# Batch 1's attention moved from beside batch 0's value and u products to beside its mix and output products, in a fused attention and two-MLP kernel

## The chip, the cores and the metric

The kernel runs on one core of a Trainium2 chip. The metric is device time in microseconds (us) of one execution. Besides TensorE (PE; its weight loads are listed as PEld) the core has VectorE (DVE), ScalarE (ACT), GpSimd (POOL) and SyncE (SP), each of which takes its instructions strictly in program order and waits for the others through semaphores. SP issues the loads and ACT the stores of the intermediate result.

## The reference, cut to what matters

For 8 batches of 576 tokens: a linear attention (8 heads of 64), then a gated MLP whose gate is mixed over tokens, then a second MLP with a convolution over tokens.

```python
q_s = softmax over the 64 of a head of q        # exp(q - max) / (sum + 1e-9)
k_s = softmax over the 576 tokens of k
kv = einsum('bhsd,bhse->bhde', k_s, v);  x = einsum('bhsd,bhde->bhse', q_s, kv)

h = gelu(x @ w_in);  u, v = halves of h
v_n = (v - mean) / sqrt(var + 1e-6) * g_ln
v_s = einsum('ts,bsd->btd', w_sg, v_n) + b_sg[None, :, None]
x1 = x + (u * v_s) @ w_out

y = (relu(x1 @ w_in2)) * sigmoid(conv over tokens) @ w_out2
```

## The kernel before, in words

The first two stages are run batch by batch in a loop `body(m, a, n)`: the gated MLP of batch m, the attention of batch a = m + 1, and the first steps of batch n = m + 2 (maximum and subtraction for its q and k). The third stage, the second MLP, follows for all batches and isn't touched. Every fp32 product is made of three: an operand is split into a high part, which ACT rounds (`hi_...`), and a low part, which DVE or POOL subtracts (`lo_...`), and PE adds high*high, high*low and low*high. Weights are split the same way, once, from a place in `plain_arena` where the raw weight was loaded, and such places are shared with tiles that are used later.

On PE the order of `body(m, a)` is: value product in four steps of d (`v_part`, 12 matmuls of 512 columns a step) with the last two `x_piece` between them, the value tail, four `u_unit` (24 matmuls of 288 columns each), four `sg_unit` (the mix over tokens, 24 matmuls and 4 of a tail), then `o_part` (the output product) with the next batch's first two `x_piece`. Among these stand the attention of batch a: five `turn_q` (transposes of q, 4 matmuls each) and five `kv_piece` (4 matmuls each).

What runs beside it, for batch m: ACT's `gelu_v`, then DVE's `moments` and `normalise` with POOL's `inverse_deviation`, ACT's `hi_vn`, POOL's `lo_vn`, and a small transfer `move_tail`; this is called the norm chain below. `u_unit(m, 2)` and `(m, 3)` reuse the banks that ACT's `gelu_u(m, 0)` and `(m, 1)` empty, and these stand behind `hi_vn(m, 0)` and `hi_vn(m, 1)` in ACT's order. In the mix, DVE's `affine`, POOL's `gate`, ACT's `hi_g` and DVE's `lo_g` follow one another for each of the four f. For batch a: ACT's `exp_q`, DVE's `sum_q` (a sum, then L1097 and a reciprocal), POOL's `scale_q`, PE's `turn_q`, ACT's `hi_q` and DVE's `lo_q` (`tile(j)`); and the subtraction of the maximum of k, ACT's `exp_k`, `kv_piece`, `finish_kv`, `hi_kv`, `lo_kv`. `max_k` reads a load of k transposed (kT), which `spread_kmax` sends through memory to all partitions.

Batch 0 has no batch before it, so its attention is `first_attention`, and `body(0, 1, 2)` follows it while weights are still being loaded and split.

## Time and profile before

| | |
|---|---|
| Times of three runs | 951.46, 952.41 and 952.91 us, median 952.41 |
| The profiled execution | 951.53 us, of which the span of the trace is 949.7 |
| Busy share of the span | PE 97%, PEld 91%, DVE 64%, ACT 40%, POOL 36% |
| Idle of PE from 28 us to 220 us | three waits, of 2.08, 1.91 and 2.67 us, the last of them ending at 56.88 |
| Chain that ended last | PE 90%, DVE 5%, DMA 1%, issue 1%, ACT 1% |

The busy share is over the whole span. The change lies in its first 125 us, and there the table of slices shows PE at 6 to 9 tenths, beside 9 for nearly all that follows; how long PE waits, and for whom, is read from the timeline of that stretch.

### The profile page before, as it was taken

Reading aid. Unit: us, or ns where it says so; the run is one execution under the profiler, and the core shown is the slowest. Engines: PE = TensorE matmul, PEld = TensorE weight load, DVE = VectorE, ACT = ScalarE, POOL = GpSimd, SP = SyncE. Lnnn points to the kernel's source line nnn. Section 1 sums busy time; section 2 is a strip of 40 time slices with the busy share of each in tenths; the row PEclk is TensorE's granted clock in tenths of the full one; section 3 lists DMA queues with packets and bytes.
Section 4 is the critical chain, followed back from the end, with each engine's and each line's share of the span. In section 5 each row is a group of like instructions: output and inputs, shape, how many; then the busy total and the mean of one; then the engine's idle time right before and its main releaser. Section 6 shows DMA issues by size and latency. Waiting matters only on the chain.

```text
span 949.7 us, 14686 instructions
## 1 busy us (share of the span) xinstructions
PE 925.5 (97%) x5980; PEld 865.6 (91%) x5980; DVE 607.9 (64%) x951; ACT 375.8 (40%) x564; POOL 345.7 (36%) x222
## 2 busy tenths in 40 slices
PE   6689999999999999999999998999999999999998
PEld 6589999899999998999999997999999989999987
DVE  6784765657747656576356797866667676667660
ACT  3561543434524434345224245533434343434331
POOL 4742634446436344464304233322232222232220
PEclk8889999999999999999999999999999999999999
DMA  9805216125062161340312302020202020200001
GB/s 316 272 20 166 91 30 189 50 75 193 12 164 92 32 190 46 80 138 12 132 53 95 110 13 73 12 77 24 78 23 73 23 72 23 82 25 18 29 23 55
DMA packets 50482, 77.84 MB, mean 82 GB/s; under 512 B 4336, under 2 KB 22768, under 8 KB 49520
## 3 DMA queue, kind: packets, MB, share of 16 engines
q1 hardware_dynamic: 45808, 67.48, 22.3%
q10 hardware_dynamic: 4608, 9.44, 2.6%
q8 instruction: 47, 0.77, 0.3%
q14 instruction: 19, 0.16, 0.1%
HBM read 56.97 MB, written 18.89 MB: 80 GB/s over the span
## 4 chain that ended last, share of the span: by engine, by line
PE 90%; DVE 5%; DMA 1%; issue 1%; ACT 1%; POOL 0%; SPq 0%; ACTq 0%; DVEq 0%
PE psum L437 54%; PE psum L429 28%; PE psum L495 4%; PE psum L578 2%; PE psum L471 2%; PE psum L530 1%; DMA plain_arena<-in_q 1%; DVE plain_arena L1291 1%; DVE split_arena L1273 1%; DVE split_arena L1409 0%; DVE plain_arena L1289 0%; PE psum L450 0%; DMA plain_arena<-in_k 0%; DVE plain_arena L1094 0%; DVE plain_arena L1105 0%
## 5 line engine op out<-in xcount | busy, mean ns | idle before, releaser
L437 PE MATMUL psum<-split_arena 128*128 128x288 f32 x4032 | 560.8, 297 | 6.2 <-ACT plain_arena L823 2.7
L437 PEld LDWEIGHTS psum<-split_arena 128*128 128x128 f32 x4032 | 547.3, 189 | 13.0 <-ACT plain_arena L823 3.1
L429 PE MATMUL psum<-split_arena 128*128 128x512 f32 x1248 | 299.1, 394 | 4.6 <-DVE split_arena L1409 2.6
L429 PEld LDWEIGHTS psum<-split_arena 128*128 128x128 f32 x1248 | 232.3, 189 | 52.1 <-DVE split_arena L1409 3.5
L1535 POOL TENSOR_TENSOR plain_arena<-plain_arena 128x576 f32<-128x576 f32 x64 | 107.8, 1684 | 281.2 <-ACT plain_arena L891 281.2
L1294 DVE SCALAR_TENSOR_TENSOR plain_arena<-plain_arena 128x576 f32<-128x576 f32 x64 | 96.2, 1503 | 2.2
L1289 DVE TENSOR_SCALAR plain_arena<-plain_arena 128x576 f32<-128x576 f32 x64 | 36.0, 563 | 90.6 <-ACT plain_arena L885 90.6
L1492 POOL TENSOR_TENSOR plain_arena<-plain_arena 128x576 f32<-128x576 f32 x32 | 46.6, 1455 | 123.3 <-DVE plain_arena L1218 123.3
L885 ACT ACTIVATE plain_arena<-psum 128x576 f32<-128x576 f32 x64 | 41.7, 651 | 105.7 <-PE psum L437 74.6
L891 ACT ACTIVATE plain_arena<-plain_arena 128x576 f32<-128x576 f32 x64 | 43.7, 682 | 42.9 <-DVE split_arena L1409 39.8
L1218 DVE SCALAR_TENSOR_TENSOR plain_arena<-psum,plain_arena 128x576 f32<-128x576 f32 x32 | 26.2, 818 | 53.7 <-PE psum L578 53.7
L1409 DVE TENSOR_TENSOR split_arena<-plain_arena,split_arena 128x576 fp32r<-128x576 f32 x64 | 53.2, 832 | 10.7 <-ACT split_arena L897 9.7
L1291 DVE SCALAR_TENSOR_TENSOR plain_arena<-plain_arena 128x576 f32<-128x576 f32 x64 | 56.0, 874 | 2.3
L1017 ACT ACTIVATE plain_arena<-psum 128x512 f32<-128x512 f32 x36 | 21.4, 595 | 87.5 <-PE psum L429 87.4
L1486 POOL TENSOR_TENSOR split_arena<-plain_arena,split_arena 128x1024 fp32r<-128x1024 f32 (+1 forms) x24 | 48.3, 2026 | 17.8 <-ACT split_arena L835 17.8
L1481 POOL TENSOR_TENSOR plain_arena<-plain_arena 128x2 f32<-128x2 f32 (+1 forms) x24 | 19.6, 818 | 89.3 <-DVE plain_arena L1191 89.3
L1456 POOL TENSOR_TENSOR plain_arena<-plain_arena 128x1024 f32<-128x1024 f32 (+1 forms) x24 | 38.4, 1618 | 35.7 <-DVE plain_arena L1085 35.7
L1461 POOL TENSOR_TENSOR plain_arena<-plain_arena 128x1024 f32<-128x1024 f32 (+1 forms) x24 | 39.6, 1652 | 27.5 <-DVE plain_arena L1100 27.4
L495 PE MATMUL psum<-plain_arena 128*128 128x130 f32 x320 | 44.7, 287 | 2.9 <-ACT plain_arena L770 2.9
L897 ACT ACTIVATE split_arena<-plain_arena 128x576 fp32r<-128x576 f32 x64 | 43.1, 674 | 8.1 <-POOL plain_arena L1535 8.1
L1225 DVE TENSOR_TENSOR split_arena<-plain_arena,split_arena 128x576 fp32r<-128x576 f32 x32 | 24.3, 758 | 33.7 <-ACT split_arena L850 33.7
L495 PEld LDWEIGHTS psum<-plain_arena 128*128 128x128 f32 x320 | 42.4, 203 | 3.0 <-ACT plain_arena L770 3.0
(81 smaller groups left out, 756.9 us busy)
## 6 DMA issues: line engine op xcount, KB each, us to landing
x_dram<-plain_arena ACTq DMA_DIRECT2D x32, 288.0 KB, 2.1
plain_arena<-x_dram SPq DMA_DIRECT2D x8, 1152.0 KB, 5.5
out_rows<-plain_arena SPq DMA_DIRECT2D x36, 256.0 KB, 2.0
plain_arena<-in_v SPq DMA_DIRECT2D x32, 256.0 KB, 3.2
plain_arena<-in_kT SPq DMA_DIRECT2D x7, 1152.0 KB, 9.2
plain_arena<-in_k SPq DMA_DIRECT2D x7, 1024.0 KB, 5.4
plain_arena<-in_q SPq DMA_DIRECT2D x7, 1024.0 KB, 5.7
plain_arena<-in_w_in SPq DMA_DIRECT2D x8, 512.0 KB, 5.6
```

The source lines that it names most:

```text
L429: mm = e.matmul(out, stat[s], mov[m], start=first and n == 0, stop=last and n == 2, skip_group_check=True)
L437: mm = e.matmul(out[:, h, 0:NH], stat[s], mov[m][:, h * NH:(h + 1) * NH], start=first and n == 0, stop=last and n == 2, skip_group_check=True)
L495: mm = e.matmul(kv_sums[:, d // 2, d % 2, 0:VW], kn[:, j, d * P:(d + 1) * P], v_place(b, j)[:, d, :], start=j == 0 and d % 2 == 0, stop=j ...
L885: e.activation(dst, main_sets[f % 2][:, :, 0:NH], ACT.Relu).then_inc(h_relu, 1)
L891: e.activation(gt[:, f % 2, :], cv[:, f % 2, :], ACT.Sigmoid).then_inc(h_gate, 1)
L897: e.activation(hg(0, par, f), gt[:, f % 2, :], ACT.Identity).then_inc(hg_hi, 1)
L1291: e.scalar_tensor_tensor(out=out, in0=h[:, 0:T], scalar=conv[:, f, 0:1], in1=out, op0=ALU.mult, op1=ALU.add).then_inc(conv_chain, 1)
L1294: e.scalar_tensor_tensor(out=out, in0=h[:, 2:T + 2], scalar=conv[:, f, 2:3], in1=out, op0=ALU.mult, op1=ALU.add).then_inc(h_conv, 1)
L1409: e.tensor_tensor(hg(1, par, f), gt[:, f % 2, :], f32(hg(0, par, f)), ALU.subtract).then_inc(hg_lo, 1)
L1486: e.tensor_tensor(vn[1][0:rows, t:t + n, :], vg[0:rows, t:t + n, :], f32(vn[0][0:rows, t:t + n, :]), ALU.subtract).then_inc(vn_lo, 1)
L1492: e.tensor_tensor(uT[:, f, :], uT[:, f, :], tmp[:, f % 2, :], ALU.mult).then_inc(gate_done, 1)
L1535: e.tensor_tensor(gt[:, f % 2, :], gt[:, f % 2, :], hp[:, f % 2, 1:T + 1], ALU.mult).then_inc(hg_full, 1)
```

## The change

In `body(0, 1, 2)` alone, PE no longer has `turn_q(1, 0)` ahead of the value tail, nor `kv_piece` and `turn_q` behind `u_unit(0, 0)` and `(0, 2)`: all ten pieces of batch 1's attention now stand behind `sg_unit(0, 1)`, `(0, 2)` and `(0, 3)`. The exponentials and sums of batch 1 move with them, behind `gelu_u` on ACT and behind `normalise` on DVE; the subtraction of k's maximum moves from DVE (`sub_second_k`) to POOL (`sub_k`). The weights of the mix (`W_SG`) are loaded and split earlier, those of the output (`W_OUT`) later, from other places: `W_SG[1]` from where `w_in` was staged, `W_OUT` from where kT lies, so that the load of batch 2's kT now waits for `lo_w_out`. The first loads of kT, q, k and v of batch 1 come in another order.

```diff
@@ places of the raw weights
-                 for f, at in ((0, UT_AT), (2, UT_AT + 1024))]
+                 for f, at in ((0, KT_AT), (2, KT_AT + 1024))]
-                for j, n, at in ((0, 2, X1_AT), (2, 2, VG_AT + 3 * F), (4, 1, BSG_AT))]
+                for j, n, at in ((0, 2, X1_AT), (2, 2, UT_AT), (4, 1, BSG_AT))]
@@ sync: load_kT
+                if isinstance(b, int) and b == 2:
+                    e.wait_ge(w_out_lo, len(W_OUT))
@@ sync: first loads
+            load_w(W_SG[2], w_sg_raw[2])
+            e.wait_ge(kv_step, NJ - 1)
+            load_w(W_SG[0], w_sg_raw[0])
             load_kT(1)
-            load_w(W_SG[2], w_sg_raw[2])
+            e.wait_ge(w_lo, 2)
+            load_w(W_SG[1], w_sg_raw[1])
+            load_q(1)
+            load_k(1)
...
             spread_kmax(1)
+            for n in range(len(W_OUT)):
+                load_w(W_OUT[n], w_out_raw[n])
@@ tensor: body
                 for f in range(FT):
                     u_unit(m, f)
-                    if f % 2 == 0:
+                    if f % 2 == 0 and not start:
                         kv_and_turn(f // 2)
                 for f in range(FT):
                     sg_unit(m, f)
-                    if f < 2:
+                    if start:
+                        if f == 1:
+                            turn_q(a, 0)
+                            kv_and_turn(0)
+                        elif f == 2:
+                            kv_and_turn(1)
+                            kv_and_turn(2)
+                        elif f == 3:
+                            kv_and_turn(3)
+                            kv_piece(a, NJ - 1)
@@ scalar: body
+                    if start and f >= 2:
+                        hi_late(W_OUT, w_out_raw, w_out_hi, f - 2)
...
+                if start:
+                    for u in range(NU):
+                        exp_q(a, u)
+                    for u in range(NU):
+                        exp_k(a, u)
@@ vector: body
+                if start:
+                    lo_w_out(0)
+                    lo_w_out(1)
+                    sum_q(a, 0)
+                    affine(m, 0)
+                    sum_q(a, 1)
+                    sum_q(a, 2)
+                    lo_g(m, 0)
+                    max_k(n, 0)
+                    affine(m, 1)
+                    tile(0)
+                    tile(1)
+                    lo_g(m, 1)
+                    max_k(n, 1)
+                    affine(m, 2)
+                    tile(2)
+                    tile(3)
+                    lo_g(m, 2)
+                    affine(m, 3)
+                    tile(4)
@@ gpsimd: body
+                if start:
+                    for u in range(NU):
+                        sub_k(a, u)
                 for f in range(FT):
                     gate(m, f)
+                    if start and f == 0:
+                        for u in range(NU):
+                            scale_q(a, u)
```

The order on DVE between the end of the first attention and batch 0's moments (`BN_STATS`), before: `lo_x(0, 3)`, the last `sum_q`, three subtractions of k's maximum (L1117), the split of `W_SG[1]` (L1266) and of `W_OUT` (L1261).

```order
L1160 TENSOR_TENSOR split_arena<-psum,split_arena 128x576
L1094 TENSOR_REDUCE plain_arena<-plain_arena 64x8
L1097 TENSOR_SCALAR plain_arena<-plain_arena 64x8
L1100 RECIPROCAL plain_arena<-plain_arena 64x8
L1117 TENSOR_TENSOR plain_arena<-plain_arena 128x1024 x2
L1117 TENSOR_TENSOR plain_arena<-plain_arena 64x512
L1266 TENSOR_TENSOR split_arena<-plain_arena,split_arena 128x1152
L1261 TENSOR_TENSOR split_arena<-plain_arena,split_arena 128x1024 x2
L1174 BN_STATS plain_arena<-plain_arena 128x6 x2
```

The same stretch now, from `lo_x(0, 0)` (L1191; L1297 splits a piece of `W_SG`, L1159 is `max_k(1, ...)`, L1123 `max_q(1, ...)`):

```order
L1191 TENSOR_TENSOR split_arena<-psum,split_arena 128x576
L1297 TENSOR_TENSOR split_arena<-plain_arena,split_arena 128x576
L1191 TENSOR_TENSOR split_arena<-psum,split_arena 128x576
L1297 TENSOR_TENSOR split_arena<-plain_arena,split_arena 128x1152
L1191 TENSOR_TENSOR split_arena<-psum,split_arena 128x576
L1159 TENSOR_REDUCE plain_arena<-plain_arena 128x2
L1191 TENSOR_TENSOR split_arena<-psum,split_arena 128x576
L1297 TENSOR_TENSOR split_arena<-plain_arena,split_arena 128x1152
L1159 TENSOR_REDUCE plain_arena<-plain_arena 128x2
L1123 TENSOR_REDUCE plain_arena<-plain_arena 128x16 x2
L1123 TENSOR_REDUCE plain_arena<-plain_arena 64x8
L1205 BN_STATS plain_arena<-plain_arena 128x6 x2
```

The sums of q, the subtractions on k and the split of `W_OUT` have left the stretch ahead of batch 0's moments; maxima of k and q, which stood further ahead, now end it, and a 576-wide split stands between the first two `lo_x`.

DVE from the last two `normalise` (L1205) on, before (L1134 is `lo_q`, L1128 `max_k(2, ...)`, L1218 the first `affine`):

```order
L1205 TENSOR_SCALAR plain_arena<-plain_arena 128x512 x2
L1205 TENSOR_SCALAR plain_arena<-plain_arena 64x512
L1134 TENSOR_TENSOR split_arena<-psum,split_arena 128x4x128
L1128 TENSOR_REDUCE plain_arena<-plain_arena 128x2
L1134 TENSOR_TENSOR split_arena<-psum,split_arena 128x4x128
L1128 TENSOR_REDUCE plain_arena<-plain_arena 128x2
L1218 SCALAR_TENSOR_TENSOR plain_arena<-psum,plain_arena 128x576
```

And now, `normalise` being L1236:

```order
L1236 TENSOR_SCALAR plain_arena<-plain_arena 128x512 x2
L1236 TENSOR_SCALAR plain_arena<-plain_arena 64x512
L1292 TENSOR_TENSOR split_arena<-plain_arena,split_arena 128x1024 x2
L1132 TENSOR_REDUCE plain_arena<-plain_arena 128x16
L1135 TENSOR_SCALAR plain_arena<-plain_arena 128x16
L1138 RECIPROCAL plain_arena<-plain_arena 128x16
L1249 SCALAR_TENSOR_TENSOR plain_arena<-psum,plain_arena 128x576
```

The two splits of `W_OUT` (L1292) and the first `sum_q` (L1132 to L1138) now stand ahead of the first `affine` (L1249).

POOL from the last weight split on, before: three `sub_q(1, ...)` (L1456), three `scale_q` (L1461), the norm chain (L1481, L1486), four gates (L1492).

```order
L1456 TENSOR_TENSOR plain_arena<-plain_arena 128x1024 x2
L1456 TENSOR_TENSOR plain_arena<-plain_arena 64x512
L1461 TENSOR_TENSOR plain_arena<-plain_arena 128x1024 x2
L1461 TENSOR_TENSOR plain_arena<-plain_arena 64x512
L1481 TENSOR_TENSOR plain_arena<-plain_arena 128x2 x2
L1486 TENSOR_TENSOR split_arena<-plain_arena,split_arena 128x1024
L1481 TENSOR_TENSOR plain_arena<-plain_arena 64x1
L1486 TENSOR_TENSOR split_arena<-plain_arena,split_arena 128x1024
L1486 TENSOR_TENSOR split_arena<-plain_arena,split_arena 64x512
L1492 TENSOR_TENSOR plain_arena<-plain_arena 128x576 x4
```

And now (L1508 is `sub_q`, L1533 and L1538 the norm chain, L1520 `sub_k`, L1544 `gate`, L1513 `scale_q`):

```order
L1508 TENSOR_TENSOR plain_arena<-plain_arena 64x512
L1533 TENSOR_TENSOR plain_arena<-plain_arena 128x2 x2
L1538 TENSOR_TENSOR split_arena<-plain_arena,split_arena 128x1024
L1533 TENSOR_TENSOR plain_arena<-plain_arena 64x1
L1538 TENSOR_TENSOR split_arena<-plain_arena,split_arena 128x1024
L1538 TENSOR_TENSOR split_arena<-plain_arena,split_arena 64x512
L1520 TENSOR_TENSOR plain_arena<-plain_arena 128x1024 x2
L1520 TENSOR_TENSOR plain_arena<-plain_arena 64x512
L1544 TENSOR_TENSOR plain_arena<-plain_arena 128x576
L1513 TENSOR_TENSOR plain_arena<-plain_arena 128x1024 x2
L1513 TENSOR_TENSOR plain_arena<-plain_arena 64x512
```

`scale_q(1, ...)` has moved from ahead of the norm chain to behind it, and three `sub_k(1, ...)` and a gate stand between.

## Rows read from the trace of the kernel before

**Rows 1.** PE's timeline, 31 to 62 us: start, duration, engine, line, operation.

```profile
31.91 4.07 PE L429 MATMUL psum<-split_arena 128*128 128x512 f32 x12
...
41.61 1.06 PE L437 MATMUL psum<-split_arena 128*128 128x288 f32 x6 [2.08 <-DVE split_arena L1160]
...
47.30 4.62 PE L429 MATMUL psum<-split_arena 128*128 128x512 f32 x12 [1.91 <-DVE split_arena L1160]
...
56.88 4.97 PE L437 MATMUL psum<-split_arena 128*128 128x288 f32 x24 [2.67 <-ACT plain_arena L823]
```

**Rows 2.** Chain of work that ended last, 77 to 122 us: start, duration.

```profile
77.28 0.53 PE psum L578 x4
77.82 0.89 PE psum L495 x8
78.71 0.44 PE psum L471 x4
...
92.54 14.38 PE psum L437 x108
...
121.78 3.18 PE psum L437 x24
```

**Rows 3.** Busy time by stretch, with granted clock (after POOL busy).

```profile
41.60:47.30 5.70, 3.79 (x18) 2.96 (x18) 4.88 (x8) 3.25 (x6) 4.90 (x4) 1.00 0.98 386
47.30:51.80 4.50, 4.50 (x13) 3.53 (x14) 4.43 (x5) 4.29 (x5) 3.25 (x2) 0.62 0.15 63
```

**Rows 4.** DVE's and POOL's timelines, narrow stretches at 49 and 64 us.

```profile
48.80 1.18 DVE L1117 TENSOR_TENSOR plain_arena<-plain_arena 128x1024 f32<-128x1024 f32 x1
...
49.90 2.06 DVE L1117 TENSOR_TENSOR plain_arena<-plain_arena 128x1024 f32<-128x1024 f32 x1
...
48.95 1.93 POOL L1461 TENSOR_TENSOR plain_arena<-plain_arena 64x512 f32<-64x512 f32 x1 [0.33 <-DVE plain_arena L1100]
...
63.87 2.44 DVE L1205 TENSOR_SCALAR plain_arena<-plain_arena 128x512 f32<-128x512 f32 x1
...
63.63 2.40 POOL L1486 TENSOR_TENSOR split_arena<-plain_arena,split_arena 128x1024 fp32r<-128x1024 f32 x1 [1.07 <-ACT split_arena L835]
```

**Rows 5.** POOL's timeline, 24 to 117 us.

```profile
24.14 9.33 POOL L1474 TENSOR_TENSOR split_arena<-plain_arena,split_arena 128x1024 fp32r<-128x1024 f32 x4
...
67.95 3.63 POOL L1486 TENSOR_TENSOR split_arena<-plain_arena,split_arena 128x1024 fp32r<-128x1024 f32 x2 [1.14 <-ACT split_arena L835]
78.83 1.42 POOL L1492 TENSOR_TENSOR plain_arena<-plain_arena 128x576 f32<-128x576 f32 x1 [7.25 <-DVE plain_arena L1218]
...
101.46 6.03 POOL L1468 TENSOR_TENSOR plain_arena<-plain_arena 128x1024 f32<-128x1024 f32 x3
...
110.37 1.91 POOL L1461 TENSOR_TENSOR plain_arena<-plain_arena 128x1024 f32<-128x1024 f32 x1 [1.87 <-DVE plain_arena L1100]
```

**Rows 6.** DVE's timeline, 28 to 101 us.

```profile
28.38 1.34 DVE L1128 TENSOR_REDUCE plain_arena<-plain_arena 128x2 f32<-128x1152 f32 x1
...
56.03 1.27 DVE L1174 BATCH_NORM_STATS2 plain_arena<-plain_arena 128x6 f32<-128x512 f32 x2
...
58.14 0.69 DVE L1134 TENSOR_TENSOR split_arena<-psum,split_arena 128x512 fp32r<-128x512 f32 x1
...
96.44 2.92 DVE L1085 TENSOR_REDUCE plain_arena<-plain_arena 128x16 f32<-128x1024 f32 x3
100.58 0.77 DVE L1242 TENSOR_TENSOR psum<-psum,split_arena 128x576 f32<-128x576 f32 x1 [1.21 <-PE psum L437]
```

**Rows 7.** ACT's timeline, 53 to 69 us.

```profile
53.60 1.28 ACT L823 ACT_TABLE_LOAD   x1
...
67.77 0.63 ACT L843 ACTIVATE plain_arena<-psum 128x576 f32<-128x576 f32 x1
```

**Rows 8.** DMA issues at 84 and 90 us: size, time from issue to landing.

```profile
plain_arena<-in_q SPq DMA_DIRECT2D x1, 1024.0 KB, 5.8
...
plain_arena<-in_kT SPq DMA_DIRECT2D x1, 1152.0 KB, 9.1
```

More of the change, by code:

```diff
@@ L939, in body @@
                 hi_x(m, DT - 2)
+                if late:
+                    exp_k(a, 2)
+                    exp_q(a, 2)
+                hi_x(m, DT - 1)
                 if start:
-                    for u in range(NU):
-                        exp_q(a, u)
-                hi_x(m, DT - 1)
+                    hi_late(W_SG, w_sg_raw, w_sg_hi[1], 1)
                 hi_x_tail(m)
@@ L983, in body @@
                         hi_w2(5)
-                if n is not None:
+                if n is not None and not start:
                     exp_q(n, 0)
@@ L1332, in tile @@
                         lo_q(a, j)
-                if a is not None and not start:
+                if a is not None and not start and not late:
                     sum_q(a, 0)
@@ L1346, in body @@
                         lo_w2(w)
-                if start:
-                    for u in range(NU):
-                        sub_second_k(u)
-                    lo_w_sg(1)
-                    lo_w_out(0)
-                    lo_w_out(1)
                 moments(m, 0)
-                tile(0)
+                if not start:
+                    tile(0)
                 sum_tail(m)
```

124 lines of the change are left out of this document (68 added, 56 removed).

## The prediction

> **What bounds the kernel now.** I read PE's waits first, then its timeline, the chain of waits, the granted clock by stretch, and last DVE's, POOL's and ACT's timelines where PE waits. From 56.88 us on PE has no wait that these views show up to 220 us; the chain runs through PE alone [rows 2]. Ahead of that PE waits three times: 2.08 us ahead of 41.61, 1.91 ahead of 47.30, 2.67 ahead of 56.88 [rows 1]. The first two are for `lo_x`, which stands on DVE behind batch 1's maxima and sums of q; the third is for batch 0's gelu on ACT, which stands behind batch 1's exponentials and the splits of `W_SG[1]` and `W_OUT`. Around them PE is slow as well: 12 matmuls of 512 columns take 4.62 us where the granted clock averages 0.62, and the first u product takes 4.97 where the same 24 matmuls take 3.18 later [rows 1 to 3]. So what there is to win is this front, and since all of PE's work behind it is unchanged, the time moves by as much as the start of batch 0's output product moves, which I call S. Before, S is 92.54: from it run 108 matmuls in 14.38 us, and batch 1's first u product starts at 121.78 [rows 2].
>
> **What goes.** Without the three waits (6.7), the slow clock behind the second (about 1.8) and `turn_q(1, 0)` (0.44), PE would reach batch 0's first u product at about 48.0 [rows 1, 2]. One new wait comes in on the way. POOL splits the four `w_in` from 24.14 in 9.33 us, to 33.47 [rows 5], and `lo_w_sg(2)`, which reads both inputs from SBUF as L1117 does, now stands between the first two `lo_x` on DVE, at 31.8. What such a subtraction does beside POOL the trace shows at 49 us: the first L1117 takes 1.18 us, the next, asked for while POOL's L1461 was waiting, takes 2.06, and that L1461, of half the size, takes 1.93 where the full size takes 1.91 [rows 4, 5]. They take turns, one whole instruction at a time. The Trainium skill says the same (SBUF — State Buffer, Who interferes with whom: such a DVE instruction and a GpSimd one that reads SBUF share a port pair, the loser is fully blocked, and reductions never contend); by it the terms below would be the same. So `lo_w_sg(2)` ends at about 34.2, the second `lo_x` at 34.9, and PE, whose first 6 matmuls of the 12 at 31.91 end near 34.4 [rows 1], loses 0.5. U products then start at 48.4.
>
> **Batch 0's norm chain.** `x_piece(0, 3)` starts where PE's idle time now begins, 39.53, plus 0.5: 40.0. Then about 1.0 for it, 0.65 for `hi_x` (an ACT operation on 576 columns, 0.63 [rows 7]) and 1.1 for the split on ACT (estimate from that, twice the width), so DVE's low split of `W_SG[1]` starts at 42.8; it and `max_k`, 1.3 each, and three `max_q`, 2.92 [rows 6], end at 48.2. The moments start there instead of at 56.03. But now POOL subtracts q's maxima beside them, 46.6 to 51.4 (two full sizes at 1.91 and a half [rows 5]), and the small operations of `moments(0, 0)` with two inputs in SBUF take turns with it: between 1.0 (they all slip in at one boundary, 50.4) and 1.9 (they wait for the end). I take 1.5, so the chain runs as if from 49.7. Its lengths are those of before, counted from 56.03 [rows 4, 5, 7], less 0.6 for the `lo_q` inside (58.14, [rows 6]): `gelu_u(0, 1)` ended at 68.40, so 11.8 on, 61.5; the last `lo_vn` at 71.58, so 14.95 on, 64.65. PE waits for `gelu_u(0, 0)` some 2.4 and for `gelu_u(0, 1)` 1.1, since no attention lies between the u products any more. The fourth ends at 61.5 + 3.2 = 64.7, two mixes of 3.18 + 0.53 [rows 2] at 72.1. Those waits cost nothing beyond what follows, because what follows is later.
>
> **The wait that takes over.** PE at 72.1 wants `turn_q(1, 0)`, hence `scale_q(1, 0)`, and that stands on POOL behind three `sub_k`, 6.03 us, and a gate, 1.42 [rows 5], all of which used to be elsewhere. From 64.65: DVE has `lo_w_out(0)` waiting since 63.6 and takes its turn first, 1.15 (L1117's size, 1.18 [rows 4]); `sub_k` 2.4, to 68.2; `lo_w_out(1)`, 1.15; `sub_k`, to 71.75; L1097 of `sum_q`, 0.1; the last `sub_k`, to 73.1; `affine(0, 0)` ended meanwhile at 73.0; gate, 74.5; another small turn of DVE, 0.1; `scale_q`, 1.91: 76.5. PE has waited 4.4. Why DVE gets the boundary: `normalise` L1205, blocked from 63.87 on by a POOL instruction that ended at 66.03, was done at 66.31, beside POOL's next [rows 4]. From 76.5 PE has five turns (0.44), five `kv_piece` (0.89) and two mixes (3.71), 14.07 in all [rows 2], and S = 90.6. In between I find no further wait: batch 2's kT is loaded only after `lo_w_out`, 69.35, and lands 9.1 later [rows 8], at 78.5; `max_k(2, 0)` and `affine(0, 1)` then end at 81.3 where PE asks at 84.7, `lo_q(1, 0)` at 82.0 where PE asks at 82.9. So S comes 1.95 earlier.
>
> **What is given back.** First the clock. The waits of 1.91 and 2.67 were each followed by a stretch at the low clock that cost 1.8 (4.97 less 3.18), the one of 2.08 was not, with 1.00 granted behind it [rows 1 to 3]. A wait of 4.4 should be: 1.8, bounds 0 and 3.5 (two such stretches). The same behind the wait of 2.4 is swallowed by the next waits. Second, batch 2's q. Its load waits for the last `turn_q(1, ...)`, which stood well ahead of S and now stands 0.9 ahead of it. It goes out at S - 0.5, its small second part at S + 0.1, each lands 5.8 later [rows 8] and a little more for two loads of v in front: S + 6.5. Then `max_q`, 2.92, three pairs of `add_x` (1.5 a pair, from 0.77 an operation) and `lo_x`, 0.7 [rows 6]: S + 14.5, while `x_piece(1, 1)` asks for it at S + 13.6 (14.38 less its own 0.8 [rows 2]). That is 0.9, bounds 0 and 2.7. Before, `max_q` ran at 96.44, S + 3.9, and hid.
>
> Number of activation table loads, stores, all of batches 1 to 7 and the second MLP: unchanged, 0.
>
> **Sum**: -1.95 + 1.8 + 0.9 = +0.75, on the profiled 951.53, so 952.3; the median of before lies 0.9 above its profiled run, so 953.1, which I round to 953.0. Within 0.2% (1.9 us, about what a measurement of this kernel can tell from no change) the change is nothing.
>
> **Rivals.**
> 1. *The stall goes elsewhere but DVE and POOL don't hold each other up much.* If the small operations slip past (t = 48.2 instead of 49.7) and the `W_OUT` splits don't delay `sub_k`, `scale_q(1, 0)` is done 3.8 us earlier, near 72.7, S falls to 86.8, and the sum is -5.7 + 1.8 + 0.9 = -3.0: 949.4. Half of this, -1.1, is as easily had. For it: POOL's and DVE's rows overlap at 101.46 with `add_x` at its full speed [rows 5, 6], so not everything contends. Against: rows 4.
> 2. *POOL wins the boundaries.* Its next instruction is always ready behind `lo_vn`. Then both `lo_w_out` wait for the end of `sub_k` (70.7), and two splits (2.3), `sum_q` with its two small steps (1.6), affine (0.8), gate and scale (3.3) follow one another: 78.8 instead of 76.5, and the sum is +3.0: 955.4. This one is slower. It decides as soon as `sub_k` runs through without a gap: its three instructions in 6.0 us. At a delay of 1.2 beyond my sum the bound is passed. For it: at 49.90 POOL, having asked first, went ahead of DVE [rows 4].
> 3. *The clock stays up, or falls only while PE waits anyway.* Then +0.75 - 1.8 = -1.05: 951.4. For it: 2.08 without a fall.
> 4. *Batch 2's q lands late*, by its upper bound: +0.75 + 1.8 = +2.5: 955.0. Kmax of batch 2 and two v loads go out in the 3 us ahead of it.
> 5. *The change doesn't do what it says*, PE's front still waits as before for q or weights: `W_SG[1]` is issued at 28.9 and wanted at 41.6, q wanted at 45.3, with 5.8 and more to land [rows 8]; against it speaks that slack.
>
> **How the numbers follow.** My forecast 0.45; rival 1, whole or half, 0.25; rival 2 0.13; rival 3 0.09; rival 4 0.06; rival 5 0.02. Faster by over 0.2%: most of rival 1 and a little of rival 3 and of mine, 0.25. Slower: rival 2, rival 4, and the upper end of mine, 0.26. Within: 0.49. Between the whole of rival 1 and rival 2 the range is 949.6 to 955.6; my forecast's own is 951.5 to 954.5.
>
> **What would show it.** In the profile after: no wait of PE from 35 us to about 48, and the first u product there at full clock (3.2 us); waits of some 2.4 and 1.1 ahead of the third and fourth; `lo_w_sg(2)` with 1.6 or more instead of 0.75; one long wait of PE for `scale_q`, 3 to 5 us, ending near 76; `sub_k` stretched to about 8.5; a low clock behind; 108 matmuls starting near 92; batch 1's first u product at 121 to 123. I am wrong if POOL and DVE run through each other there, if the long wait is under 2 us, or if a new one stands between S and batch 1's value product over 3 us.

## The result and the profile after

The changed kernel takes 958.94 us (median of 6 runs, 957.16 to 960.45), the kernel before 952.64 (6 runs, 951.46 to 954.03): a ratio of 1.0065, 95% interval 1.005 to 1.0079. It is slower by 6.3 us. I had forecast 953.0 within 949.6 to 955.6, so the range missed it.

PE's timeline of the changed kernel, 34 to 132 us, with start, duration, engine, line, and the idle time ahead in brackets:

```profile
34.99 1.66 PE L436 MATMUL psum<-split_arena 128*128 128x512 f32 x6 [1.26 <-DVE split_arena L1191]
...
48.08 6.55 PE L444 MATMUL psum<-split_arena 128*128 128x288 f32 x48
57.41 12.50 PE L444 MATMUL psum<-split_arena 128*128 128x288 f32 x72 [2.77 <-ACT plain_arena L859]
...
78.45 1.08 PE L478 MATMUL psum<-plain_arena 128*128 128x128 f32 x4 [4.28 <-POOL plain_arena L1513]
...
95.04 10.63 PE L444 MATMUL psum<-split_arena 128*128 128x288 f32 x78
107.50 6.16 PE L444 MATMUL psum<-split_arena 128*128 128x288 f32 x30 [1.83 <-DVE plain_arena L1280]
...
128.33 3.35 PE L444 MATMUL psum<-split_arena 128*128 128x288 f32 x24
```

The front answers to [rows 1] much as foretold: u products start at 48.08 (I said 48.4), the first 48 matmuls at full clock. Then come three waits: for gelu on ACT (2.77; I said 2.4), for `scale_q(1, 0)` on POOL (4.28; I said 4.4), and for the first `add_x` on DVE (1.83; I said 0.9). That the second is of the size foretold is luck: both its ends are some 2 us later than I had them (74.17 and 78.45, not 72.1 and 76.5). Behind each the clock is down. These are rows of busy time by stretch for PE alone: stretch, its length, PE busy (count), granted clock, DMA share, GB/s.

```profile
57.40:66.50 9.10, 9.10 (x48) 0.67 0.06 14
...
74.10:84.00 9.90, 5.62 (x27) 0.66 0.37 143
...
107.50:113.50 6.00, 5.88 (x30) 0.72 0.45 173
```

The account, by equal rows of the timelines: the output product of batch 0 (S) starts at 95.04, where the same view of the kernel before has 92.38; batch 1's first u product at 128.33 where it has 121.61. So 2.7 us are lost up to S, 4.1 between S and that product, and the rest of the spans' difference (957.7 less 949.7), 1.3, behind it. These are single profiles: the one of the kernel before lies 1.1 under its median, the changed kernel's 0.6 over, so 1.7 of the 8.0 are not in the 6.3 of the medians. Another profile of the same front, of the control e12 below, has S at 94.00.

**Up to S.** What follows PE's long wait took 95.04 less 78.45, 16.6 us, instead of 14.07: 2.5 of clock. The wait itself ended at 78.45, not 76.5, because of what the narrow timelines of DVE and POOL show:

```profile
65.19 5.26 DVE L1292 TENSOR_TENSOR split_arena<-plain_arena,split_arena 128x1024 fp32r<-128x1024 f32 x1 [4.66 <-ACT split_arena L894]
...
64.63 2.38 POOL L1520 TENSOR_TENSOR plain_arena<-plain_arena 128x1024 f32<-128x1024 f32 x1
...
66.98 4.62 POOL L1520 TENSOR_TENSOR plain_arena<-plain_arena 128x1024 f32<-128x1024 f32 x2
```

`lo_w_out(0)` asks at 65.19, while the first `sub_k` runs. That ends at 66.98, and POOL's second goes ahead: DVE gets its turn only at 69.3, ahead of the third and smallest, and is done at 70.45.

**Behind S.** Batch 2's q goes out at 94.58 with k, v and batch 3's kT right behind it (95.80 to 97.77). On DVE `max_q` waits for q, and the third `add_x` waits for a store of batch 0's rows to land, since its place in `x1` is still being read:

```profile
102.93 2.93 DVE L1123 TENSOR_REDUCE plain_arena<-plain_arena 128x16 f32<-128x1024 f32 x3 [4.38 <-DMA plain_arena<-in_q]
...
111.12 0.76 DVE L1280 TENSOR_TENSOR plain_arena<-psum,split_arena 128x576 f32<-128x576 f32 x1 [1.54 <-DMA x_dram<-plain_arena]
```

PE waits 1.83, and the 30 matmuls behind run 6.0 us, to 113.50, where 30 of the 108 in 14.38 [rows 2] would take 4.0. The two sum to 3.8 of the 4.1. The late store (3.6 us to land) hides behind the slow clock here; the experiments bring it out.

**Behind batch 1's first u product** the last 1.3 is clock. Far down PE waits the same time for the same thing in both kernels, and only the changed one's profile has slower rows behind it, a little in the first and most in the second (before, then after):

```profile
577.61 1.66 PE L429 MATMUL psum<-split_arena 128*128 128x512 f32 x6 [1.97 <-DVE split_arena L1409]
579.11 3.61 PE L437 MATMUL psum<-split_arena 128*128 128x288 f32 x24
```
```profile
584.35 1.87 PE L436 MATMUL psum<-split_arena 128*128 128x512 f32 x6 [1.98 <-DVE split_arena L1461]
586.01 4.71 PE L444 MATMUL psum<-split_arena 128*128 128x288 f32 x24
```

### The profile page after: what moved, and what is told of

It is laid out like the page before. It is cut to its first block, busy times and chain, and to the rows that moved or that the text cites. A ratio compares the mean times of both kernels' runs of the same rounds, so it can differ in the third digit from the quotient of the medians.

```text
span 957.7 us, 14686 instructions
## 1 busy us (share of the span) xinstructions
PE 928.5 (97%) x5980; PEld 869.3 (91%) x5980; DVE 614.8 (64%) x948; ACT 375.3 (39%) x564; POOL 351.4 (37%) x225
## 4 chain that ended last, share of the span: by engine, by line
PE 88%; DVE 7%; DMA 2%; issue 1%; POOL 1%; ACT 1%; SPq 0%; ACTq 0%; DVEq 0%
PE psum L444 52%; PE psum L436 28%; PE psum L502 3%; PE psum L478 2%; PE psum L585 2%; PE psum L537 1%; DVE plain_arena L1123 1%; DMA plain_arena<-in_q 1%; DVE plain_arena L1322 1%; DVE split_arena L1304 1%; DVE plain_arena L1205 1%; DVE split_arena L1461 0%; DVE plain_arena L1320 0%; DMA plain_arena<-in_k 0%; PE psum L457 0%
## 5 line engine op out<-in xcount | busy, mean ns | idle before, releaser
L1544 POOL TENSOR_TENSOR plain_arena<-plain_arena 128x576 f32<-128x576 f32 x32 | 46.4, 1451 | 118.7 <-DVE plain_arena L1249 118.7
L1461 DVE TENSOR_TENSOR split_arena<-plain_arena,split_arena 128x576 fp32r<-128x576 f32 x64 | 53.2, 832 | 10.9 <-ACT split_arena L913 10.0
L1249 DVE SCALAR_TENSOR_TENSOR plain_arena<-psum,plain_arena 128x576 f32<-128x576 f32 x32 | 26.1, 815 | 47.4 <-PE psum L585 47.4
L1508 POOL TENSOR_TENSOR plain_arena<-plain_arena 128x1024 f32<-128x1024 f32 (+1 forms) x24 | 38.4, 1618 | 49.0 <-DVE plain_arena L1123 49.0
L1538 POOL TENSOR_TENSOR split_arena<-plain_arena,split_arena 128x1024 fp32r<-128x1024 f32 (+1 forms) x24 | 48.2, 2024 | 17.8 <-ACT split_arena L851 17.8
L814 ACT ACTIVATE split_arena<-psum 128x576 fp32r<-128x576 f32 x32 | 20.9, 652 | 74.5 <-PE psum L444 46.1
L1513 POOL TENSOR_TENSOR plain_arena<-plain_arena 128x1024 f32<-128x1024 f32 (+1 forms) x24 | 39.1, 1636 | 29.6 <-DVE plain_arena L1138 29.6
L1533 POOL TENSOR_TENSOR plain_arena<-plain_arena 128x2 f32<-128x2 f32 (+1 forms) x24 | 19.6, 817 | 79.2 <-DVE plain_arena L1222 79.2
```

The costliest lines, as they stand in the source:

```text
L1461: e.tensor_tensor(hg(1, par, f), gt[:, f % 2, :], f32(hg(0, par, f)), ALU.subtract).then_inc(hg_lo, 1)
L1538: e.tensor_tensor(vn[1][0:rows, t:t + n, :], vg[0:rows, t:t + n, :], f32(vn[0][0:rows, t:t + n, :]), ALU.subtract).then_inc(vn_lo, 1)
L1544: e.tensor_tensor(uT[:, f, :], uT[:, f, :], tmp[:, f % 2, :], ALU.mult).then_inc(gate_done, 1)
```

## The experiments

Sixteen kernels, edits of the changed kernel but for one control. U1 is the start of batch 1's first u product in the profile, and the turn is the start of batch 1's first `turn_q` on PE, 78.45 in the changed kernel. The port theory says that a DVE instruction with both inputs in SBUF and a POOL instruction hold each other up, one whole instruction at a time. The ratios are to the kernel before, on the same chip.

| kernel | median us | ratio, 95% interval | S | U1 |
|---|---|---|---|---|
| before | 952.64 | | 92.38 | 121.61 |
| changed | 958.94 | 1.005 to 1.0079 | 95.04 | 128.33 |
| e1_turn4_early | 960.73 | 1.0071 to 1.0097 | 94.89 | 130.43 |
| e2_wout_behind_affine | 956.87 | 1.0035 to 1.0059 | 93.50 | 126.44 |
| e3_keep_busy | 962.82 | 1.0098 to 1.0133 | 92.26 | 128.17 |
| e4_kv_first | 956.38 | 1.0034 to 1.0058 | 92.15 | 126.23 |
| e5_kT_behind_stores | 956.29 | 1.0024 to 1.0049 | 94.94 | 126.42 |
| e6_q_early_kT_late | 956.47 | 1.0028 to 1.0053 | 95.73 | 126.24 |
| e7_scale_first | 958.52 | 1.0051 to 1.0076 | 93.85 | 128.50 |
| e8_all | 956.12 | 1.0024 to 1.0051 | 96.94 | 127.05 |
| e9_reordered | 956.29 | 1.0036 to 1.0061 | 94.44 | 126.43 |
| e10_three | 956.08 | 1.0022 to 1.0047 | 90.96 | 124.96 |
| e11_busy_kT_late | 961.57 | 1.0088 to 1.0118 | 92.29 | 126.17 |
| e12_before_kT_late | 953.03 | 0.9997 to 1.0015 | 94.00 | 123.22 |
| e13_q_first | 956.58 | 1.0029 to 1.0054 | 95.69 | 125.44 |
| e14_all_v_first | 950.45 | 0.996 to 0.9982 | 88.51 | 119.39 |
| e15_two_waits | 956.02 | 1.0025 to 1.005 | 95.20 | 126.14 |
| e16_short_sub_k | 954.40 | 1.0009 to 1.003 | 89.12 | 124.89 |

Each interval is some 0.13% wide to either side, so that a difference of 2 us between two of these kernels is at the edge of what the medians tell. S and U1 are of one profile each, and differ by 1.6 us between the kernel before and e12, whose edit acts only later: PE there waits 3.68 instead of 2.08 ahead of 42.08, and 4.27 instead of 2.67 ahead of 57.35. The places where PE waits are told by the rows.

### What makes the first turn late: DVE and POOL

**Splits of `W_OUT` moved behind.** On DVE:

```diff
-                    lo_w_out(0)
-                    lo_w_out(1)
                     sum_q(a, 0)
                     affine(m, 0)
+                    lo_w_out(0)
+                    lo_w_out(1)
```

> On DVE the two low splits of W_OUT stand behind sum_q(1, 0) and the first affine instead of ahead of them. Port theory (each W_OUT split has to wait for a boundary between POOL's subtractions, and the gate and scale_q stand behind both): sum_q and affine are done while or right behind sub_k, which runs to 71.6 at the latest, the gate starts there instead of at 75.05, PE's turn at 75.3 instead of 78.45, and the time falls by about 3 us, to 956. Since the wait shrinks to 1 us or so, the low clock behind it may go too: up to 2.6 more, 953.3. Rival (POOL's own work sets the date of scale_q, the splits only fill its shadow): the gate stays within 0.5 of 75.05 and the time stays at 958.9.

Measured: 956.87, the turn at 77.05. Half of what the port theory asked for: `sub_k` runs through in 6.00, the gate starts at 71.75, but then each split gets in ahead of POOL once. POOL's timeline of this kernel:

```profile
71.75 2.31 POOL L1544 TENSOR_TENSOR plain_arena<-plain_arena 128x576 f32<-128x576 f32 x1 [1.41 <-DVE plain_arena L1249]
74.03 2.88 POOL L1513 TENSOR_TENSOR plain_arena<-plain_arena 128x1024 f32<-128x1024 f32 x1
```

The gate takes 2.31, not 1.42 [rows 5], the scaling 2.88, not 1.9. I had moved the collision, not removed it.

**`sub_k` shortened.** The three subtractions for batch 1 work on 8 of 512 columns, the rest is left out.

```diff
+                w = 8 if isinstance(b, int) and b == 1 else D
-                e.tensor_tensor(kn[0:rows, t:t + n, :], ...
+                e.tensor_tensor(kn[0:rows, t:t + n, 0:w], ...
```

> POOL's three subtractions of k's maxima for batch 1 work on 8 columns instead of 512 (the rest of k is exponentiated unshifted, so this leaves out nearly all of that subtraction). If the port between DVE and POOL is what made the first turn late: both W_OUT splits take 1.15 instead of 5.26 and 2.31, sum_q starts at 70.9 behind the exponentials instead of 72.6, the gate at 72.6, scale_q is done at 75.8 instead of 78.4, and 2.5 us are gained, if the store and q waits leave them; the third of them at least: 956.5 to 958. If the chain exponentials, sum_q, affine, gate sets the date by itself, the turn stays within 0.5 of 78.45.

Measured: 954.40, 4.5 us less, and more of a gain than the 956.5 to 958 that the port theory asked for. The first rows are of DVE and POOL, the last of PE:

```profile
63.63 1.89 DVE L1292 TENSOR_TENSOR split_arena<-plain_arena,split_arena 128x1024 fp32r<-128x1024 f32 x1 [3.33 <-ACT split_arena L894]
66.83 1.23 DVE L1292 TENSOR_TENSOR split_arena<-plain_arena,split_arena 128x1024 fp32r<-128x1024 f32 x1 [1.31 <-ACT split_arena L894]
...
64.41 1.53 POOL L1521 TENSOR_TENSOR plain_arena<-plain_arena 128x16 f32<-128x16 f32 x3
...
75.08 0.63 PE L478 MATMUL psum<-plain_arena 128*128 128x128 f32 x4 [2.45 <-POOL plain_arena L1513]
```

The splits take 1.89 (waiting for the end of `lo_vn`) and 1.23, and the turn comes at 75.08. A kernel told below, e15, has the same front and the whole `sub_k`. There `lo_w_out(0)` asked at 63.53, as I had predicted (63.6), with `lo_vn` still running, and was passed over twice:

```profile
63.53 6.69 DVE L1298 TENSOR_TENSOR split_arena<-plain_arena,split_arena 128x1024 fp32r<-128x1024 f32 x1 [3.24 <-ACT split_arena L900]
...
63.14 1.28 POOL L1544 TENSOR_TENSOR split_arena<-plain_arena,split_arena 64x512 fp32r<-64x512 f32 x1
64.39 4.75 POOL L1526 TENSOR_TENSOR plain_arena<-plain_arena 128x1024 f32<-128x1024 f32 x2
```

Its turn came at 78.22. So POOL's `sub_k` and its collision with the splits cost 3.1 us of the turn (78.22 less 75.08). That S comes 5.9 us earlier in e16 than in the changed kernel has a second cause: behind its wait of 2.45 no slow clock follows, and from the turn to S it takes 14.04 us, the 14.07 of my sum, where the changed kernel takes 16.6. Of this 2.5 is gone again at U1, where PE waits 2.59 for `add_x` and 1.79 for `lo_x`.

**Scaling ahead of the gate**, on top of e2:

```diff
+                if start:
+                    scale_q(a, 0)
                 for f in range(FT):
                     gate(m, f)
                     if start and f == 0:
-                        for u in range(NU):
-                            scale_q(a, u)
+                        scale_q(a, 1)
+                        scale_q(a, 2)
```

> The second experiment (both W_OUT splits behind sum_q and the first affine) and on POOL scale_q(1, 0) ahead of the first gate. There the gate took 2.31 instead of 1.4 and scale_q 2.88 instead of 1.9, each behind one W_OUT split of DVE, and PE's turn came at 77.05. Port theory: scale_q now starts when sum_q is done, 71.1, runs in 1.9, at most one split of 1.15 goes ahead of it, so PE's turn comes at 73.0 to 74.2: 2.9 to 4 us earlier than in the second experiment, PE's wait shrinks to 0.5 to 1.6, and the slow clock behind it (1.9) goes. Time 951 to 953, if the waits ahead of batch 1's value product don't grow; they have grown each time that the output product started earlier (2.2 + 0.6 at 92.2, 1.7 + 2.9 at 92.3), so rather 954. Rival (the exponentials or batch 2's loads hold it up): turn at 76 or later.

Measured: 958.52. The turn comes at 73.24, just as the port theory said, with 0.42 of wait; all is lost again at 84.50, where PE waits 4.69 for `lo_q`, which stands on DVE behind batch 2's `max_k`, whose kT now goes out at 76.59 since `w_out_lo` is later. The wait of `max_k` for kT is only 0.76 of it; the rest is DVE's own work ahead, the `W_OUT` splits (4.84 for the two) and the sums of q.

### What is in the wait, and the clock behind it

**kv products first.** On PE:

```diff
                         if f == 1:
+                            kv_piece(a, 0)
+                            kv_piece(a, 1)
                             turn_q(a, 0)
-                            kv_and_turn(0)
+                            turn_q(a, 1)
                         elif f == 2:
-                            kv_and_turn(1)
+                            turn_q(a, 2)
```

> Two of batch 1's five kv products stand ahead of its first turn of q, in PE's longest wait, and the later ones move up accordingly. If the wait for scale_q is pure waiting (my account of the wait), 1.8 us of useful work move into it: the wait shrinks from 4.28 to 2.5 or, where the clock also stays up behind the shorter wait, the gain is 1.8 + 2.6. So 957.1, at best 954.5. Rival (what follows the turn, batch 2's kT, max_k and the affines, is next in line and takes the gain away): unchanged, 958.9.

Measured: 956.38, between its two figures; the wait is 3.66, S 92.15, 2.9 earlier. Of this 0.8 is lost again behind S (PE waits 2.17 for `add_x` instead of 1.83, then 0.59 for `lo_x`).

**Filling the waits with matmuls** that nobody reads, 18 and 30 of 288 columns:

```diff
+            def keep_busy(n):
+                for _ in range(n):
+                    e.matmul(psum[:, 5, 0:NH], win[0][:, 0, 0:P], win[0][:, 0, 0:NH],
+                             start=True, stop=True, skip_group_check=True)
...
+                    if f == 1 and start:
+                        keep_busy(18)
...
+                            keep_busy(30)
```

> Adds 18 matmuls of 288 columns behind batch 0's second u product and 30 ahead of batch 1's first turn of q, on data already there and into a bank that nobody reads: they fill the two waits and change no result. Clock theory (the slow stretches behind the waits of 2.77 and 4.28 are made by PE's idling): no granted clock of 0.50 behind either, the output product of batch 0 starts 2.6 to 4.6 us earlier, the time is 954.5 to 956.5. Rival (the waits and nothing but the waits cost the time, or the added work just takes the place of the idling and runs over): between 0 and +1 us.

Measured: 962.82, against both expectations; all that is added is this idle work. The clock theory is right up to S: 1.00 is granted throughout and S is 92.26, 2.8 earlier. But all of it is lost at the end of the output product, where PE waits 1.66 for `add_x` and then 2.88 for `lo_x`, the latter behind the late store. Further waits of 1.64 and 1.53 for the same `lo_x` appear at 240.67 and 368.75, where the changed kernel has none. The same with batch 3's kT held back:

> Filling PE's two long waits with work that nobody reads kept the clock up and moved the output product from 95.1 to 92.4, but the time got worse, since the store of batch 0's rows was waited for. The same filling with batch 3's kT behind the stores. Compared with the changed kernel plus the late kT alone (956.3): if the clock's price is 2.6 to 2.8 and only the store hid it, 953.5 to 954; if max_q's wait takes it (q lands when it lands), 955.5 to 956.3.

Measured: 961.57; at U1 it is level with e5 (126.17 and 126.42), so `max_q` (2.03 of wait and a slow stretch) and the store (0.55) took the gain there, as the second expectation had it, and 5.5 us more are lost later, 3.7 of them in two such waits at 238.80 and 367.35. Why filling PE early makes later batches' stores late I have not found.

### Behind S: q, the stores and the queue of loads

**The last turn and batch 2's q load earlier.** On PE and SP:

```diff
                             kv_and_turn(2)
+                            turn_q(a, NJ - 1)
                         elif f == 3:
-                            kv_and_turn(3)
+                            kv_piece(a, 3)
...
                     spread_kmax(n)
+                    if isinstance(m, int) and m == 0:
+                        load_q(n)
                     load_v(n, 0)
                     load_v(n, 1)
-                    load_q(n)
```

> The last of batch 1's five turns of q stands ahead of the fourth mix instead of behind it, and batch 2's q load goes out ahead of the two v loads that stood in front of it. Theory A (batch 2's q, loaded late, puts max_q, add_x and lo_x behind PE's need, and the slow clock follows that wait): the q load goes out at about 85.5 instead of 94.6, max_q is past on DVE before the output product needs it, the wait of 1.83 ahead of 107.50 and the low clock behind it go, and the stretch from the start of batch 0's output product to batch 1's first u product falls from 33.3 to about 29.3: 4.1 us less, near 954.9. Theory B (the wait is made by the store of batch 0's rows, 3.6 us to land beside k, v and kT): it shrinks by half at most, 2 us less or nothing, 957 to 959. Whatever stands ahead of 95 us stays as it is in both.

Measured: 960.73. Theory A fell. Theory B had the right thing in the store, but not the time, which lies above both. The wait for `max_q` is gone (102 matmuls run through), and a longer one stands six matmuls on. PE, then DVE:

```profile
94.89 13.82 PE L447 MATMUL psum<-split_arena 128*128 128x288 f32 x102
113.11 1.22 PE L447 MATMUL psum<-split_arena 128*128 128x288 f32 x6 [4.40 <-DVE split_arena L1195]
```
```profile
111.63 0.76 DVE L1284 TENSOR_TENSOR plain_arena<-psum,split_arena 128x576 f32<-128x576 f32 x1 [4.79 <-DMA x_dram<-plain_arena]
```

A store took 6.9 us to land, beside k, v and kT, where the kernel before needs 2.1. There the last load is out at 90.49, and in the 8 us from 100 us the DMA engines are busy 0.29 of the time; in e1 all of it (1.07 in the view of the same 8 us).

**kT of batch 3 behind the stores.** On SP, in `load_kT`:

```diff
+                if isinstance(b, int) and b == 3:
+                    e.wait_ge(x1_out[1], 32)
```

> One thing changes: the load of batch 3's kT, 1152 KB, issued at 97.77 behind batch 2's q, k and v, waits until batch 0's output rows are stored. Theory (the pile of loads that starts at 94.6 keeps the first store from landing: 3.6 us instead of 2.1 in the changed kernel, 6.9 with the q load ahead): the store lands in 2.1 to 2.5 again, and the wait ahead of the last add_x on DVE goes. By itself this is worth little here, 0 to 1 us, since PE still waits 1.83 for the first add_x behind max_q and the slow clock behind it hides the store: 958 to 959. Rival (the store's delay comes from k and q, not from kT): still 3 us or more to land.

Measured: 956.29, and every store of batch 0 lands in 2.1: the rival falls, and the gain is larger than I said. At U1 it is 1.9; the rest is that its clock stayed up at 582 us. Nearly all of the 1.9 is clock as well. PE still waits 1.46 and 0.21, but the matmuls behind run at full clock:

```profile
107.03 3.45 PE L446 MATMUL psum<-split_arena 128*128 128x288 f32 x24 [1.46 <-DVE plain_arena L1282]
```

PE asks for the last `lo_x` at 110.48 here, and in the changed kernel, behind the late store, it ends only at 112.5; so with the store late PE would have waited instead. Whether the clock stayed up because of the edit is not shown. The control:

> A control on the kernel before the change: batch 3's kT behind batch 0's stores, nothing else. There the kT goes out at 90.5, the pile is down by 101 and the stores land in 2.1, so no change is expected (952.5, within 0.2%). If it gets faster by 1 us or more too, the 2.65 that the same edit gained on the changed kernel isn't the change's own loss.

Measured: 953.03, no clear difference (the interval holds 1), stores 2.1 with and without. So the pile of loads on the stores is of the change's making: it moved the pile's start from 84.4 to 94.6.

Both together, in two forms; the second has q also ahead of `spread_kmax`:

> The first experiment (last turn of q ahead of the fourth mix, batch 2's q load ahead of two v loads), which removed the wait for max_q but came out 1.8 us slower than the changed kernel because the store of batch 0's first rows took 6.9 us to land, and with it the load of batch 3's kT held back until batch 0's rows are stored. Theory (two waits stand in line there, max_q behind q's load and the store behind the pile of loads; whoever removes one meets the other): now both go, no wait of PE over 0.3 between the start of batch 0's output product at 95 and batch 1's first u product, that stretch is 29.3 as before the change, the low clock behind it is gone, and the time is 4 us below the changed kernel, 954.9. Rival (something third stands behind them, k's load for sub_k or the maxima of k): 957 or more.

> The changed kernel with nothing touched ahead of the output product but the place of the last turn of q; batch 2's q load goes out behind it, ahead of the spreading of k's maxima, and batch 3's kT waits for batch 0's stores. If the loss behind the start of the output product is those two waits and the clock behind them: start at 95.1 to 95.8 as before this edit, no wait up to batch 1's first u product at 124.4 to 125, 954.5 to 955.2. If a third thing stands there, 956 and more.

Measured: 956.47 and 956.02, U1 at 126.24 and 126.14. e6 ends between its two expectations, e15 at the second (U1 was to be at 125 at most by the first). No wait for `max_q` is left, but the store still takes 3.4 and 3.8 us, now beside k (out at 96.0 and 98.8), and PE waits 0.95 and 1.38 for `lo_x`. An earlier q brings the `add_x` forward and so the store into what remains of the pile.

### Putting it together

> Three single edits that each gained on the changed kernel, together: W_OUT splits behind sum_q and affine (2.1 gained), two kv products ahead of the first turn of q (2.6), batch 3's kT behind batch 0's stores (2.65). If they act at different places (turn date, content of the wait, store) they add up, less what one wait can't be shortened twice: turn at 77.05 with 1.8 of work moved ahead, wait 2.5, output product at 90.7 to 91.5, then only max_q's wait (1.5 to 2.5) left: 952 to 953, about the kernel before. If the wait for max_q grows by what the product starts earlier, since q's load hangs on kmax and not on PE, 954 to 955.

Measured: 956.08. S is 90.96, near the 90.5 that the gains of e2, e4 and e5 add up to; the wait for `max_q` grows to 3.09, since q goes out at 90.49 by kmax's queue and lands at its own time. So it is the second branch, and 1 us above even that.

> The three edits that gained alone (W_OUT splits behind sum_q and affine, two kv products ahead of the first turn, batch 3's kT behind batch 0's stores) with the last turn of q ahead of the fourth mix and batch 2's q load ahead of the spreading of k's maxima on SP's queue. If the remaining loss is the wait for max_q: q goes out near 86, lands by 92, max_q runs at 95 behind the last lo_g and hides; the output product starts at 91 and runs through; batch 1's first u product at 120.4 to 121 where the kernel before has 121.78: 951 to 952, level with or just ahead of the kernel before. If the kmax detour, now later, or the store takes its place, 954 to 956.

Measured: 956.58. q ahead of kmax goes out only at 89.54, since PE's last turn waits 3.01 for `lo_q`, which stands on DVE behind `max_k` and an `affine`. The theory falls, but what took its place is DVE's row ahead of S (95.69), not the kmax detour or the store that the rival named, and the time is 0.6 above the rival's range too. From S on the kernel runs almost through (0.19 of wait).

> All of it together: q's scaling ahead of the gate, W_OUT splits behind sum_q and affine, two kv products ahead of the first turn, the last turn and batch 2's q load early, batch 3's kT behind batch 0's stores. By the theory PE's long wait is under 1 us, the output product starts near 89 to 90 (turn ready 73.5; 14.07 less 1.8 for the two kv products, plus at most 1 of clock), nothing waits between there and batch 1's value product, and batch 1's first u product stands near 119, where the kernel before has 121.78: 949 to 951, faster than both. Rival (DVE's row of work between the mixes and the output product can't follow: kT of batch 2 for its maxima, max_q, add_x): 953 to 956.

Measured: 956.12, the rival's time. The turn comes at 73.79 without a wait; then PE waits 5.81 for `lo_q`, behind the same work of DVE as in e7 (`max_k` waits 1.05 for kT). Its successor puts DVE's row in this order, and ACT's and POOL's to match:

```diff
+                    sum_q(a, 0)
+                    affine(m, 0)
+                    sum_q(a, 1)
+                    lo_w_out(0)
+                    sum_q(a, 2)
+                    lo_w_out(1)
+                    affine(m, 1)
+                    tile(0)
+                    tile(1)
+                    lo_g(m, 0)
+                    tile(2)
+                    max_k(n, 0)
+                    tile(3)
+                    max_k(n, 1)
```

> The combined version stalled anew: PE waited 5.81 ahead of 84.36 for the low split of batch 1's first turned q, which stood on DVE behind batch 2's maxima of k, and these behind batch 2's kT, which came late since its load waits for both W_OUT splits. Here DVE takes the splits of batch 1's q tiles ahead of those maxima, both maxima together, sum_q(1, 1) ahead of the W_OUT splits; ACT takes the copies of the q tiles one place earlier; POOL scales two thirds of q ahead of the first gate. If that order was the cause, no wait of PE over 1 us stands between the first turn at 73.8 and the output product, which starts at 88 to 90, and batch 1's first u product is near 119 (before the change: 121.78): 948 to 951. If DVE has no room there at all (W_OUT splits 2.3, sums 3.8, q splits 3.2, maxima 2.7, affines 3.2, lo_g 2.1 in 16 us and each one that reads SBUF twice beside POOL's scale_q), it comes to 953 to 956 again.

Measured: 956.29. The waits for `lo_q` shrink to 1.09, but PE stands 4.45 for v, which is on SP's queue behind kT:

```profile
84.74 2.07 PE L507 MATMUL psum<-plain_arena 128*128 128x130 f32 x8 [4.45 <-DMA plain_arena<-in_v]
```

The last kernel adds two edits on SP:

```diff
                     move_tail(m)
-                    load_kT(n)
                     load_v(m + 1, 2)
                     load_v(m + 1, 3)
+                    load_kT(n)
...
+                    if isinstance(m, int) and m == 0:
+                        load_q(n)
                     spread_kmax(n)
```

> The reordered version, with batch 1's v tiles 2 and 3 ahead of batch 2's kT on SP's queue (PE waited 4.45 for v there) and batch 2's q ahead of the spreading of k's maxima. If these two orders were what it fell back on, the first turn stays at 73.8, no wait over 1 us follows, the output product starts at 88 to 90, batch 1's first u product at 117 to 119: 947 to 950, faster than the kernel before. If DVE or kT of batch 2 (out at 78, in at 83.7) is what holds PE, 953 to 956.

Measured: 950.45, interval 0.996 to 0.9982: faster than the kernel before by 2.0 us and than the changed kernel by 8.5. It is just short of what I expected (947 to 950, U1 at 117 to 119, no wait over 1 us). PE's timeline:

```profile
74.28 1.03 PE L483 MATMUL psum<-plain_arena 128*128 128x128 f32 x8
...
79.94 0.66 PE L483 MATMUL psum<-plain_arena 128*128 128x128 f32 x4 [0.90 <-DVE split_arena L1174]
...
88.51 1.85 PE L449 MATMUL psum<-split_arena 128*128 128x288 f32 x12 [0.25 <-DVE plain_arena L1258]
91.53 13.18 PE L449 MATMUL psum<-split_arena 128*128 128x288 f32 x96 [1.17 <-DVE split_arena L1265]
...
119.39 3.35 PE L449 MATMUL psum<-split_arena 128*128 128x288 f32 x24
```

q goes out at 82.79, all other loads by 92.00 but batch 3's kT, held back to 107.82; `max_q` ends at 98.2, and no store takes over 2.3 us. By itself the earlier turn gained nothing (e7, 958.52) and the mended loads 2.7 to 2.9 (e5, e15); which of this kernel's edits it could do without I did not try, nor what such edits of the queues would give the kernel before, apart from e12's, which gives nothing there. So that the moved attention itself is worth the 2.0 us is not shown.

## Why the prediction was wrong

- **The front**: right. u products at 48.08 (48.4), `lo_w_sg(2)` blocked by POOL's weight splits (2.82; "1.6 or more"), gelu waits of 2.77 (2.4) and, in e1, where the clock stays up, 0.71 (1.1). One wait there was larger than I had it: 1.26 ahead of 34.99 (0.5).
- **"From 64.65: DVE has `lo_w_out(0)` waiting since 63.6 and takes its turn first": this step failed.** In e15 it waited since 63.53 and was passed over at 64.39 and at 66.74. The turn comes at 78.2 to 78.6 in every kernel with this order, not at 76.5: 1.95 in the sum. What was wrong is who goes first at a boundary, not how long each takes: the second split ended at 72.7 instead of 69.35, and the sum of q, the `affine`, the gate and the scaling follow it. That is rival 2's time (78.8), if not its sign: `sub_k` had a gap, 6.97 and not 6.0. I had settled the order of two engines by one row, a `normalise` that had waited for a POOL instruction [rows 4]; the same rows also show POOL going ahead.
- **The clock behind the long wait**: mechanism right, size 2.5 where I took 1.8 (bounds 0 and 3.5), and 0 in e16. That a slow stretch at the front would be swallowed was right too: its cost differs by 2.7 us between profiles, and the turn by 0.4. What the term lacks is a slow stretch behind the *next* wait: 2.0.
- **"That is 0.9, bounds 0 and 2.7": the term for batch 2's q** was mis-sized, and its account too narrow. PE waited 1.83; with the clock behind it, 3.8. I priced q alone, and never asked what k, v and kT, which follow it on the queue, would do to the stores of batch 0's rows: I had put stores among what is unchanged, at 0. Their number is unchanged, their time to land is not. In the changed kernel the slow clock hides it; in e1, with the wait for `max_q` gone, it is 4.4 us of wait, the largest behind S.
- **The rest**: 1.3 of the profile's difference is the clock at 584 us, which differs from profile to profile (below).

The sum by these steps, up to U1: -1.95 + 1.95 (turn) + 2.5 + 4.1 = +6.6; measured 6.7. Each of the three terms came out larger than I had put it, so the range, made of rivals taken one at a time, couldn't hold it: rival 2's price and rival 4 came together, the latter beyond its bound.

## What to carry to other kernels

A transfer that starts later by the change delays not only who waits for it but every other transfer that now falls beside it: list the stores too, and the places that they keep occupied. Where two engines block each other instruction by instruction, price the order in which neither is favoured, or measure it. Once a front is moved up, each queue behind it (DVE's row, SP's issues) has to be put in the new order of need before anything of it is seen: e7, e8 and e9 had the turn 4.7 to 5.2 us earlier, yet e7 came out at the changed kernel's time and e8 and e9 at e5's, which has no earlier turn, until in e14 the last queue was right.

## What was unexpected in the hardware

- **Who is let in.** A DVE split that asked during a full-size POOL instruction was passed over at each boundary where POOL's next one was of full size (64.39, 66.74 in e15; 66.98 in the changed kernel), and got in ahead of the third, of half the size. In e2 it got in between a gate and a scaling. The Trainium skill (SBUF — State Buffer, Who interferes with whom) has the loser fully blocked, and the trace agrees: a split that takes 1.23 in e16 takes 5.26 in the changed kernel and 6.69 in e15; by what rule one of them wins is shown by none of these rows.
- **The clock falls behind one and the same wait in some profiles and not in others.** Ahead of the third u product 14 profiles of kernels with the same program up to there have a wait of 2.77 or 2.78. In four of them (e1, e8, e9, e10) nothing falls, in eight the 72 matmuls behind take 11.1 to 11.4 us, and in two (changed, e5) 12.5 and 12.6, where 72 take 9.85 at full clock. Where nothing falls PE waits once more, 0.7 ahead of the fourth product, as in e1:

```profile
57.11 3.44 PE L447 MATMUL psum<-split_arena 128*128 128x288 f32 x24 [2.77 <-ACT plain_arena L863]
61.26 6.66 PE L447 MATMUL psum<-split_arena 128*128 128x288 f32 x48 [0.71 <-ACT plain_arena L863]
```

From the third product's start to the end of the 72 matmuls (the third and fourth product and the first mix) these four take 10.8 us, the others 11.1 to 12.6. Behind the wait of 1.97 or so near 580 us the six matmuls take 1.65 to 2.88. So the price of one wait's clock, here 0 to 2.7 in matmul time and 0 to 1.8 in PE's progress, is known only as a range, and a part of the difference between two single profiles is nothing but this.
- **PE kept busy with idle matmuls** held the clock at 1.00 up to S and still made the kernel slower (962.82 against 958.94), in part by waits in later batches whose cause stays open.
